# Attention and two gated layers on one core: split factors kept in DRAM, attention one step earlier, another order of copies and casts, stores by halves

## What is computed

```python
kv  = einsum('bhsd,bhse->bhde', k, v)          # batch 8, heads 8, seq 576, head_dim 64
o   = einsum('bhsd,bhde->bhse', q, kv)
x   = o / sqrt(mean(o*o, -1) + 1e-6) * g_norm  # then [4608 tokens, 512]
h   = sigmoid(x @ w_gate) * (x @ w_val)        # d_ff 1536
y   = h @ w_out                                # 512
z   = y @ w_in                                 # d_ff 2048
g   = where(z >= 1, z, where(z <= -1, 0, (z + 1)**2 / 4))
out = g @ w_out2                               # 512
```

## Time and profile before

| | us |
|---|---|
| median of 3 runs | 1839.04 |
| lowest and highest | 1836.62, 1839.80 |
| the profiled execution | 1838.85 |
| its span, first to last instruction | 1837.1 |
| mean granted TensorE clock | 0.967 of full |

### The profile page before, as it was taken

One profiled execution on the slowest core, in us unless ns is written; L12 is line 12 of the kernel. 1 busy time (PEld: TensorE's weight loads), 2 busy tenths in 40 slices (PEclk: granted clock), 3 DMA queues, 4 the chain that ended last, 5 costly groups with the idle time before them and its releaser, 6 DMA issues.

```text
span 1837.1 us, 31582 instructions
## 1 busy us (share of the span) xinstructions
PE 1719.0 (94%) x12526; PEld 1664.0 (91%) x12526; DVE 1216.0 (66%) x1734; ACT 887.3 (48%) x1620; POOL 194.0 (11%) x254
## 2 busy tenths in 40 slices
PE   6899999998899999799999979999999699999999
PEld 5798888987899999799999979999999599999999
DVE  3566655566666556687777877777777686766774
ACT  3565544564444345444444545555555454444443
POOL 4300000002544400110000330000000100000000
PEclk8999999998999999999999989999999899999999
DMA  6423333413465633444434333333334553544451
GB/s 209 160 97 122 136 127 109 136 52 119 158 202 198 202 123 113 160 141 143 143 129 143 136 137 129 130 130 130 130 130 162 176 174 117 157 118 127 133 141 38
DMA packets 189714, 253.18 MB, mean 138 GB/s; under 512 B 30912, under 2 KB 121024, under 8 KB 189568
## 3 DMA queue, kind: packets, MB, share of 16 engines
q1 hardware_dynamic: 177744, 207.65, 33.7%
q0 software_dynamic: 11824, 43.52, 7.4%
HBM read 143.92 MB, written 107.22 MB: 137 GB/s over the span
## 4 chain that ended last, share of the span: by engine, by line
PE 75%; DVE 11%; DMA 5%; ACT 5%; issue 4%; POOL 0%; SPq 0%; ACTq 0%; DVEq 0%
PE x L1414 13%; PE x L1416 12%; PE x L1415 12%; PE y L1414 7%; PE y L1416 7%; PE y L1415 7%; DVE t_lo L996 2%; PE m L1434 2%; PE z L1414 2%; PE z L1416 2%; PE z L1415 2%; DMA h_scratch<-gate 2%; PE h L1414 2%; PE h L1415 1%; PE h L1416 1%
## 5 line engine op out<-in xcount | busy, mean ns | idle before, releaser
L1414 PE MATMUL x<-t_hi,v_lo 128*128 128x288 f32 x1664 | 509.7, 306 | 39.3 <-ACT kept L857 20.0
L1415 PE MATMUL x<-t_lo,v_hi 128*128 128x288 f32 x1664 | 495.9, 298 | 0.0
L1416 PE MATMUL x<-t_hi,v_hi 128*128 128x288 f32 x1664 | 495.0, 297 | 0.0
L1414 PEld LDWEIGHTS x<-t_hi,v_lo 128*128 128x128 f32 x1664 | 316.4, 190 | 58.1 <-ACT kept L857 26.7
L1416 PEld LDWEIGHTS x<-t_hi,v_hi 128*128 128x128 f32 x1664 | 317.8, 191 | 0.0
L1415 PEld LDWEIGHTS x<-t_lo,v_hi 128*128 128x128 f32 x1664 | 317.5, 191 | 0.2
L1414 PE MATMUL y<-t_hi,v_lo 128*128 128x288 f32 x832 | 255.8, 307 | 41.0 <-DVE t_lo L996 12.1
L1415 PE MATMUL y<-t_lo,v_hi 128*128 128x288 f32 x832 | 249.7, 300 | 0.0
L1416 PE MATMUL y<-t_hi,v_hi 128*128 128x288 f32 x832 | 249.0, 299 | 0.0
L1414 PEld LDWEIGHTS y<-t_hi,v_lo 128*128 128x128 f32 x832 | 160.3, 193 | 50.2 <-issue 14.1
L1414 PE MATMUL x<-v_hi,t_lo 128*128 128x256 f32 x576 | 163.5, 284 | 0.9 <-ACT o_kept L966 0.9
(11 more groups left out here) (180 smaller groups left out, 3609.6 us busy)
## 6 DMA issues: line engine op xcount, KB each, us to landing
g_scratch<-c_tile SPq DMA_DIRECT2D x128, 288.0 KB, 2.4
gq<-g_scratch SPq DMA_DIRECT2D x64, 512.0 KB, 5.9
h_scratch<-gate SPq DMA_DIRECT2D x96, 288.0 KB, 2.1
hq<-h_scratch SPq DMA_DIRECT2D x32, 864.0 KB, 5.1
stage<-w_in POOLq DMA_DIRECT2D x68, 256.0 KB, 4.6
kv_ring<-kv_in SPq DMA_DIRECT2D x30, 512.0 KB, 3.8
fold_scratch<-stage POOLq DMA_DIRECT2D x14, 896.0 KB, 5.6
x_scratch<-xo SPq DMA_DIRECT2D x16, 576.0 KB, 2.8
```

Of the source, the lines that this page charges most:

```text
L1414: nc.tensor.matmul(dst, s_lo, m_hi, start=start, stop=False, skip_group_check=True)
L1415: nc.tensor.matmul(dst, s_hi, m_lo, start=False, stop=False, skip_group_check=True)
L1416: return nc.tensor.matmul(dst, s_hi, m_hi, start=False, stop=stop, skip_group_check=True)
```

## The change

Four things are edited together.

1. A fold task is now split when it is made. ACT casts it into `fold_hi`, DVE subtracts in place in `stage`, and POOL stores both parts to DRAM (2 x 0.9 MB). B and D then load both parts straight into `v_hi` and `v_lo` by POOL's queue (`load_b`, `load_d`); the 21 read-back tasks and their casts and subtractions are gone. ACT may cast the next fold only when the stores of the folds before it have landed, since `fold_hi` is one buffer.
2. Attention moves one step forward in the block: heads in steps 4, 5, 0, 1 (before 5, 0, 1, 2), `spread` in step 3 at four separate places (before step 4), kv chunks in steps 2 and 3 (before 3 and 4). At the start, the lo parts of the first two weight tasks are made by POOL (`split_low`) instead of DVE, and TensorE does 14 and 16 idle passes (before 4).
3. The order of copies, casts, sums and subtractions on ACT and DVE changes in all stages: weight casts stand before the `u2_kept` copy and their subtractions at the end of DVE's step; in C the square of a step stands after the `u3_kept` copy, and the last maximum (`finish`) one step later; sums get buffers of their own (`c_t1`, `c_t2`, `c_t4`, `t3_first`, `t4_first`, `t_late`). In B each half product waits for its own bank. The slots of the split inputs are shifted so that the first items of the next stage find theirs free, and the four quarters of h for B's first block are loaded at step 92 (before: three at step 94, the last after 95).
4. h is stored in two DMAs per step, one per half (`store_h0`, `store_h1`), each with its own semaphore.

```diff
+SECOND_SETS = {40: 0, 43: 1, 44: 2, 45: 3, 49: 4, 50: 5}
+FOLDS = {k: i for i, k in enumerate((51, 53, 55, 57, 61, 63, 67, 69, 73, 75, 79, 81, 85, 87))}
...
 # SP, step k of A
+                if k:
+                    store_h0(k - 1)
...
+                if k:
+                    store_h1(k - 1)
+                if s == 3 and b + 1 < B:
+                    store_x(b + 1, 0)
+                    store_x(b + 1, 1)
+                if k == A_STEPS - 4:
...
+                    for x in range(4):
+                        sp.dma_start(hq[x][:], h_dram[...]).then_inc(hq_loaded[x], 16)
...
 # POOL
             def store_fold(task):
-                pool.wait_ge(stage_summed, summed_count(task))
...
+                pool.wait_ge(v_ready, task + 1)
+                low = stage[:, task % 2, :, :].bitcast(f32r)
+                for dram, part in zip(fold1_dram if task < FOLD2_TASK else fold2_dram, (fold_hi[:], low)):
...
+                    pool.dma_start(dram[:, :, j, :].rearrange("x p n -> p x n"), part).then_inc(fold_stored[task % 2], 16)
...
+            def load_factor(drams, quad, first, pieces, loaded):
+                for ring, dram in ((v_hi, drams[0]), (v_lo, drams[1])):
+                    for base, at, count in pieces:
+                        pool.dma_start(ring[:, base:base + count, :], dram[quad, :, first + at:first + at + count, :]).then_inc(loaded, 16)
...
+            def load_b(i):
+                if i >= 2:
+                    pool.wait_ge(p_done[3], A_STEPS - A_SETS + min(i - 1, 4))
+                load_factor(fold1_dram, QUAD[ORDER[i]], 0, b_pieces(i), b_loaded[i])
...
+            def load_d(x):
+                pool.wait_ge(p_done[3], D0 - C_SETS + (4 * x + 3) // SEVEN + 1)
+                load_factor(fold2_dram, QUAD_D[ORDER_D[x // 2]], 4 * (x % 2), d_pieces(x), d_loaded[x])
...
+            def split_low(task):
+                pool.wait_ge(v_hi_done, task + 1)
...
+                nc.gpsimd.tensor_tensor(v_lo[:, base:base + count, :], stage[:, task % 2, first:first + count, :],
+                                        v_hi[:, base:base + count, :].bitcast(f32), ALU.subtract).then_inc(v_ready, 1)
...
 # ACT
+                if is_fold(task):
...
+                    for earlier in range(max(FOLD1_TASK, task - 2), task):
+                        act.wait_ge(fold_stored[earlier % 2], 32 * len(range(FOLD1_TASK + earlier % 2, earlier + 1, 2)))
+                    nc.scalar.copy(fold_hi[:], stage[:, task % 2, :, :]).then_inc(v_hi_done, 1)
...
 # ACT, step k of A: p1 copy, sigmoid, root, items, then
+                if k in SECOND_SETS:
+                    split_weights(A2_TASK + SECOND_SETS[k])
+                if k in FOLDS:
+                    split_weights(FOLD1_TASK + FOLDS[k])
...
                 if k < A_STEPS:
                     act.wait_ge(p_done[6], k + 1)
                     reach(act, c12_ready, k - 1)
                     nc.scalar.copy(kept[:, 1 + k % 2, :], X[k % 2][:, 0:C]).then_inc(u2_kept, 1)
...
 # DVE, step k of C
+                if k >= 2:
+                    finish(k - 2)
...
-                if k:
-                    dve.wait_ge(square_ready, k)
-                    tile = c_tile[:, (k - 1) % 3, :, :]
-                    nc.vector.tensor_tensor(tile, tile, c_sq[:], ALU.max).then_inc(g_ready, 1)
-                if C_STEPS - 6 <= k < C_STEPS:
-                    for task in ((0,), (1, 2), (3, 4), (5, 6), (7,), (8, 9))[k - (C_STEPS - 6)]:
-                        split_weights(D_TASK + task)
...
 # TensorE, step k
+                if number == 6 and heads_of(k):
+                    heads(*heads_of(k))
+                if number == 1 and mean_of(k):
+                    mean_square(*mean_of(k))
...
+                if b + 1 < B and s == 3 and number in (1, 4, 3, 7):
+                    spread(b + 1, (1, 4, 3, 7).index(number))
...
                     if u == 0 and j % 4 == 0:
-                        pe.wait_ge(v_ready, split_of(D_TASK) + 2 * i + j // 4 + 1)
+                        pe.wait_ge(d_loaded[2 * i + j // 4], 32 * len(d_pieces(2 * i + j // 4)))
```

More of the change, by code:

```diff
@@ L18 @@
 CONSTANTS = 6 + 2 * (P // D)
-WARM_START, WARM_COPY = 10, 4
+WARM_START, WARM_COPY, WARM_ROOT = 10, 14, 16
 C = S // 2
@@ L44, with parts @@
 QUAD_D = {1: 0, 5: 4, 6: 5, 2: 2, 7: 1, 3: 3, 4: 6}
-A1_TASK, A2_TASK, FOLD1_TASK, FOLD2_TASK, B_TASK, C_TASK, D_TASK, TASKS = 0, 6, 12, 18, 26, 33, 41, 55
-def split_of(task):
-    return task if task < FOLD1_TASK else task - (B_TASK - FOLD1_TASK)
+A1_TASK, A2_TASK, FOLD1_TASK, FOLD2_TASK, C_TASK, TASKS = 0, 6, 12, 18, 26, 34
+B_LOADS, D_LOADS = SEVEN, 2 * SEVEN
+SECOND_SETS = {40: 0, 43: 1, 44: 2, 45: 3, 49: 4, 50: 5}
+FOLDS = {k: i for i, k in enumerate((51, 53, 55, 57, 61, 63, 67, 69, 73, 75, 79, 81, 85, 87))}
 def is_fold(task):
[L55 to L88, removed]
+    return FOLD1_TASK <= task < C_TASK
+def parts(base, count):
     base %= CHUNKS
@@ L221, in program @@
         fold_stored = [sem(f"fold_stored{i}") for i in range(2)]
+        b_loaded = [sem(f"b_loaded{i}") for i in range(B_LOADS)]
+        d_loaded = [sem(f"d_loaded{x}") for x in range(D_LOADS)]
         v_hi_done = sem("v_hi_done")
@@ L776, in _ @@
                 square_heads(0, c)
-            for c in range(1, K):
-                scale_heads(0, c)
+            scale_heads(0, 1)
+            root(0)
             split_weights(0)
-            root(0)
+            split_inverse(0)
+            scale_heads(0, 2)
+            scale_heads(0, 3)
             split_weights(1)
-            split_inverse(0)
-            for i in range(5):
+            for i in range(4):
                 split_item(0, i)
@@ L787, in _ @@
                 b, s = divmod(k, A_SETS)
-                c = (s + 1) % A_SETS
-                n = b + 2 if s == 5 else b + 1
-                normal = 2 <= n < B and c < K
-                if normal:
-                    split_query(n, c)
-                if s == 3 and b + 1 < B:
-                    root(b + 1)
+                more = b + 1 < A_BLOCKS
                 if k < A_STEPS:
@@ L821, in _ @@
                     nc.scalar.copy(kept[:, 1 + k % 2, :], X[k % 2][:, 0:C]).then_inc(u2_kept, 1)
-                if normal:
-                    scale_heads(n, c)
+                if s == 4 and more:
+                    split_item(b + 1, 1)
+                if s == 5 and more:
+                    split_item(b + 1, 2)
+                    split_item(b + 1, 3)
+                if s == 0 and b < A_BLOCKS:
+                    split_item(b, 5)
+                    split_item(b, 6)
+                if k == A_STEPS - 1:
+                    split_b_item(1)
+                if k == 1:
+                    square_heads(1, 2)
+                    scale_heads(1, 2)
+                if heads_of(k):
+                    square_heads(*heads_of(k))
+                    split_square(*heads_of(k))
+                if k == A_STEPS:
+                    split_b_item(2)
                 if k:
@@ L1596, in _, with b_product @@
                     attention(k, 7)
-            def b_product(b, i, number, banks, start):
+            def b_product(b, i, number, banks, start, freed, count, whole):
                 if b == 0:
-                    pe.wait_ge(v_ready, split_of(B_TASK) + i + 1)
+                    pe.wait_ge(b_loaded[i], 32 * len(b_pieces(i)))
                 for hh in range(2):
@@ L1605, in b_product @@
                     for m in range(2):
+                        if hh == 0:
+                            reach(pe, freed, count if whole else count + m - 1)
                         part = slice(P * m, P * (m + 1))
```

661 lines of the change are left out of this document (347 added, 314 removed).

## The result

The change gives 1788.55 us (median of 4 runs, 1786.39 to 1791.29) where before took 1838.71 (4 runs): ratio 0.973, interval 0.971 to 0.975. It is faster by 50 us. The forecast was 1720, from 1697 to 1765, so the sign was right and the size was not. The profiled execution took 1786.39.

The account below looks back on a forecast made before the run. The prediction took TensorE as the bound, with 170 us lost between its matmuls that the change could touch, beside the start. Gains per stretch summed to 119 us: 1838.85 - 119 = 1720 us, range 1697 to 1765.

Parts of the forecast that it names:

- The losses in A that the prediction named: Steps 1-6, blocks 1-5, block 6 and block 7 of A: TensorE's waits shrink, gaining 7.5, 30, 8.5 and 7.5 us.
- rival D: The order in A was not the cause: blocks 1-15 keep their losses, stage changes still gain; 1774 us, chance 0.09.
- Rival B: In A the clock still falls once a block, from the 16-row spreads, not the wait; 1748 us, chance 0.25.
- A to B: Change of stage from A to B: h loaded at step 92, items spread over steps 95 and 96; gain 13 us.
- product 7 waits 17.4 - 11.2 - 4.7 = 1.5 us. There are 8 such pairs: Blocks 8-15: a fold's cast waits 2.3 us for stores, delaying product 7; 10 us cost, net gain 8.
- quarters loaded at step 92 (3.5 MB, 9 us at 391 GB/s): End of A: the loads of h for B's first block, issued at step 92, take 9 us.
- at 391, load 13 lands some 24 us after product 7: Start of D: at 391 GB/s factor load 13 lands when asked for; at 300 GB/s it is 10 us late.
- C to D gain of 21: Change from C to D: 29.3 us lost shrinks to 8.5, stalls of 7.5 and 1 for the clock.
- Rival C: Transfers bind: D's loads come 10 us late, fold stores 2 us later each; 1746 us, chance 0.13.
- Its stage is loaded a block earlier: B to C: one weight split where four stood, loaded earlier, shrinks the 10.1 us wait; 3 left, gain 11.5 us.
- the 40.6 of the working: Start: first product at 40.6 us (before 38.1), yet fewer waits after it; gain to step 1 of 5 us.
- the POOL subtraction as a brake: Start: POOL's 5.1 us subtractions and DVE's work exclude each other, so DVE waits up to 5 and 1.5 us.

Follow-up runs that it names:

- e1: Kernel after the change, with a second place for the first part of a fold, so casts wait for the stores of the fold two before: 1764.97 us.
- e2: Kernel after the change, with POOL's loads of B's 5th to 7th factors held until the four loads of h have landed: 1778.41 us.
- e6: Kernel after the change, with the four loads of h issued one per step at steps 92 to 95 instead of all at 92: 1783.64 us.
- e10: Kernel after the change, with e1, e2, e7 and e8 combined, B's loads held from the third, hq and gq loads spread, first folds a step later: 1735.53 us.
- e16: e10 with the folds back at their old steps (51, 53, 55, 57): 1731.45 us, ratio 0.942.
- e7: Kernel after the change, with C's casts of factors 5, 6, 7 in steps 1, 2 and 4 instead of 0, 1 and 2: 1782.31 us.
- e11: Kernel after the change, with the lo parts of the first two weight tasks made on DVE again, none by POOL: 1787.72 us.
- e12: Kernel after the change, with the idle passes of before (10, 4 and none instead of 10, 14 and 16): 1788.65 us.
- e5: Kernel after the change, without loading the factors' second parts ahead of B and in D (22 MB less, result incomplete): 1769.86 us.
- e8: Kernel after the change, with POOL's loads of D's factors two at a time: 1784.26 us.
- e13: Kernel after the change, with D's first four gq loads one ahead of each of four g stores in C's last block: 1781.85 us.
- e3: Kernel after the change, with POOL's loads of D's factors one at a time, each issued when the one before has landed: 1804.03 us.

## Why the prediction was wrong

**Right.** The losses in A that the prediction named went: steps 1-6, blocks 1-5, 6 and 7 gave 54.3 us of 53.5 forecast, and blocks 1-5 lose 9.6 us where 7.8 were left. That the sum is so near is in part luck: block 6 gave 3.0 more than forecast, blocks 1-5 gave 1.8 less. So rival D is out. No run separates the earlier attention from the new order of copies and casts, so which of them gave what is argued from the waits that went. Rival B is out too, at least for spreads as they stand now: at the place behind the spreads where the granted clock was 0.57 with 35 matmuls in 8 us it is now

```profile
132.00:140.00 8.00, 8.00 (x60) 7.55 (x59) 5.87 (x12) 4.05 (x10) 0.00 (x0) 1.00 0.44 168
```

The spreads are still there, 2.5 to 3.4 us apart (before: 1.7 to 3.1), and the wait of 1.3 us is not: at this spacing and without the wait they do not bring the clock down. B and C were better than forecast by 1.3 and 3.4. A to B gave 14.0 of 13, but the move of the loads to step 92, made for this gain, cost 20.35 us in step 95.

**Wrong: "product 7 waits 17.4 - 11.2 - 4.7 = 1.5 us. There are 8 such pairs".** The mechanism was right, and ACT did wait eight times for a store. The cost was not: 10 us were put down, and the waits for stores cost 27.5. At the five later pairs ACT waited 3.2 to 3.3 us where 2.3 were forecast, PE 2.0 to 2.1 where 1.5, and the term left out the clock that falls behind such a wait, 1.7 us each. I had written of waits "of 1.8 to 2.2 us elsewhere" that brought falls, as an argument against rival B, and did not apply it to my own 1.5. The three that follow each other cost less together, as forecast (8.4 us), but one of them alone cost 6.7. The 3.8 us of the first fold, behind POOL's sums, stood in no term. e1 takes the waits for stores away and measures them: 25.9 us in A2, 23.6 in the whole.

**Wrong: "quarters loaded at step 92 (3.5 MB, 9 us at 391 GB/s)".** The sum asked when the loads would land and not what stands behind them on SP's queue. POOL loads three factors of 1.57 MB beside them; a load of h took up to 20.7 us to landing, and the gate stores behind them waited too: 20.35 us that no term had. e2 shows the share of the loads of h alone, e6 that of the factors, and e10 and e16 that without both the stall is gone.

**Wrong: "at 391, load 13 lands some 24 us after product 7" and a C to D gain of 21.** Rival C had the transfers 10 us late, in D's factors. They were not late. What waited was the small g stores and the gq loads beside them, ahead of D, and with them PE: 12.2 us that no term had. The stalls at D's start together were of the size forecast, 7.7 us where 7.5 stood, but by luck: product 5 waited 4.4 us for its item where 1.4 were put down, product 6 waited 3.3 for its copy where 5.3 were. The clock was not: "1 for the clock" became 6.9, as it was at 0.50 for 5.2, 3.3 and 5.3 us behind these three waits. Another wait of 2.7 us fell into D's first unit, which took 43.5 us in place of 40.3. The prediction cited the Trainium skill (DMA: Bandwidth & Descriptors, Issuing engines are not separate DMA queues), that DMAs of all issuing queues share the same engines, so that POOL's loads take from SP's stores. The traces agree, and more than the sum allowed: one rate of 391 GB/s does not say how long a store of 288 KB waits. They took up to 15.9 us to landing.

**Wrong in size: B to C.** "Its stage is loaded a block earlier" does not hold for the factors split in C's first steps. The one of step 0 (`C_TASK + 5`) is loaded from 1016.5 on, and its sums are ready at 1026.5; the new place of the cast, ahead of the copy, made that a wait of 6.8 us and 2.9 for the clock. e7 shows 3.9 us of it.

**The start.** Product 1 stood at 35.60, earlier than the 40.6 of the working, but step 0 then took the time back: waits of 1.9 for a kv chunk and 1.9 and 1.0 for scaled heads, and a clock of 0.51 and 0.68 in two stretches of 4.2 and 5.4 us. What I said of the POOL subtraction as a brake is not borne out: e11 changed nothing. The second set of idle passes is 16 more and not 12, since before had none there; e12 shows that neither set matters.

Open: how the 12 us of bytes at C to D could be had without the doubled read (e5 leaves the second parts out of the result), why stalls of 2.5, 4.7 and 3.7 us stay around D's start even there, and what each of the earlier attention, the order in A, and the edits in B and C gave by itself.

## What to carry to other kernels

A wait of about 2 us on TensorE cost nearly twice its length here, since the clock fell behind most of them: count each one with its clock. Before moving a large load to an earlier place, list the small stores that follow it on the same queue and what other queues load in the same time; who waits for those stores is next. Work that is moved from engines to the DMA is free only where the DMA has room: around both changes of stage it had little or none.

## What the runs showed of the hardware

- A DMA issue is not cheap when the transfers are backed up: one hq load took SP 11.5 us to issue and one g store 10.3, where others took 0.37 and 0.32; what stood behind it on the queue was issued later. The view of SP's issues of hq (shortest, median and longest in ns, then the start of the first and the last):

```profile
L462 SPq DMA_DIRECT2D hq<-h_scratch x4: 371/1727/11483, 712.2 to 716.5; - x4
```

- The granted clock stayed at 1.00 (2.4 GHz) for 0.5 to 1.5 us after each of the seven waits of 2.0 to 2.1 us in A, and only then went to 0.50 (1.2 GHz), for 3.4 us. This is not certain: over the kernel after and the ten runs that keep these waits (e2 to e8, e11 to e13) it fell behind 68 of 77. One of the nine without a fall, in e8, with 39 matmuls in the 5 us that follow:

```profile
560.81 0.40 PE L1498 MATMUL x<-t_hi,v_lo 128*128 128x288 f32 x1 [2.02 <-ACT kept L879]
```

```profile
561.00:566.00 5.00, 5.00 (x39) 5.00 (x39) 4.74 (x7) 2.70 (x7) 2.18 (x3) 1.00 0.45 148
```

- After the waits of 6.8 and 12.2 us the clock was at 0.50 from the first matmul on, for 5.9 and 5.2 us.
- More transfers in flight meant longer single ones, and more rate only up to a point. From 1350 to 1410 us, with one factor of D at a time (e3), two (e8) and no limit (after), the DMA moved 254, 331 and 319 GB/s, and the median time to landing of a load into `v_hi` was 4.6, 6.2 and 7.3 us. One at a time starved D by 24 us; two at a time did not cost PE a wait for them.
